# The rest of the keys' P is split into a rounded and a low part in the attention of a fused attention and two feed-forward layers

## The reference

```python
q_rot, k_rot = rotate(q), rotate(k)                      # [4, 8, 576, 64]
scores = (1 / sqrt(64)) * q_rot @ k_rot^T
attn = exp(scores - max); attn = attn / (sum(attn) + 1e-9)
x = (attn @ v) as [2304, 512]
h = x @ w_in;   x = (h - tanh(h)) @ w_out                # 512 -> 2048 -> 512
h = x @ w_in2;  out = (h * sigmoid(h)) @ w_out2
```

## Time and profile before

| | |
|---|---|
| median of three runs | 1110.88 us |
| the profiled execution's own time | 1111.94 us |
| its span, first to last instruction | 1110.1 us |
| mean granted TensorE clock | 1.000 |
| TensorE busy | 1075.9 us, 97% of the span |
| VectorE busy | 443.0 us, 40% |
| ScalarE busy | 419.5 us, 38% |
| GpSimd busy | 282.6 us, 25% |
| attention | up to 301 us of the span |
| feed-forward layers | from 301 us to the end |

### The profile page before, as it was taken

The page is one execution under the profiler, slowest core; times in us unless marked ns, Lnnn a source line. Parts: engine busy times, 40 slices in busy tenths (PEclk is TensorE's granted clock), DMA queues, the critical chain, the costliest instruction groups (busy, mean ns, idle before and its releaser), DMA issues.

```text
span 1110.1 us, 16519 instructions
## 1 busy us (share of the span) xinstructions
PE 1075.9 (97%) x6608; PEld 987.7 (89%) x6608; DVE 443.0 (40%) x712; ACT 419.5 (38%) x775; POOL 282.6 (25%) x121
## 2 busy tenths in 40 slices
PE   2899999999999999999999999999999999999998
PEld 1778888888899999999999999899999999899997
DVE  5566666666253323223232333623223232322322
ACT  1567686676722323223232322323223232232322
POOL 5776978873551000000000015700000000000000
PEclk9999999999999999999999999999999999999999
DMA  5344446532152000000000004200000000000000
GB/s 182 133 154 146 133 127 217 162 102 71 29 168 76 1 1 0 0 0 0 0 0 0 0 0 151 76 1 29 0 0 28 0 28 0 0 28 0 29 0 28
DMA packets 36331, 58.35 MB, mean 53 GB/s; under 512 B 15680, under 2 KB 17984, under 8 KB 34368
## 3 DMA queue, kind: packets, MB, share of 16 engines
q1 hardware_dynamic: 36288, 57.78, 16.0%
HBM read 48.37 MB, written 4.79 MB: 48 GB/s over the span
## 4 chain that ended last, share of the span: by engine, by line
PE 89%; POOL 5%; DVE 2%; DMA 1%; ACT 1%; issue 1%; SPq 0%; ACTq 0%; POOLq 0%; DVEq 0%
PE ps L597 35%; PE ps L616 18%; PE ps L611 17%; PE ps L535 6%; PE ps L501 4%; PE ps L466 2%; PE ps L530 2%; PE ps L527 1%; PE ps L503 1%; PE ps L493 1%; POOL wout_l L399 1%; POOL hl L379 1%; POOL win_l L399 1%; DVE hm L777 1%; POOL raw L374 1%
## 5 line engine op out<-in xcount | busy, mean ns | idle before, releaser
L597 PE MATMUL ps<-xs_h,win_l 128*128 128x384 f32 x768 | 258.6, 337 | 1.4 <-DVE xs_l L834 1.4
L597 PE MATMUL ps<-xs_h,win_h 128*128 128x384 f32 x768 | 257.6, 335 | 0.0
L597 PE MATMUL ps<-xs_l,win_h 128*128 128x384 f32 x768 | 257.1, 335 | 0.0
L742 ACT ACTIVATE g_h<-ps 128x384 fp32r<-128x384 f32 x192 | 94.5, 492 | 306.3 <-PE ps L616 135.1
L736 ACT ACTIVATE act<-ps 128x384 f32<-128x384 f32 x192 | 94.5, 492 | 247.6 <-PE ps L597 247.4
L597 PEld LDWEIGHTS ps<-xs_h,win_l 128*128 128x128 f32 x768 | 144.2, 188 | 7.5 <-issue 3.9
L597 PEld LDWEIGHTS ps<-xs_l,win_h 128*128 128x128 f32 x768 | 144.2, 188 | 3.5
L597 PEld LDWEIGHTS ps<-xs_h,win_h 128*128 128x128 f32 x768 | 144.1, 188 | 0.0
L777 DVE TENSOR_REDUCE hm<-ps 128x2 f32<-128x576 f32 x144 | 108.5, 756 | 79.8 <-PE ps L466 77.9
L399 POOL TENSOR_TENSOR win_l<-w_stage,win_h 128x2048 fp32r<-128x2048 f32 x8 | 39.6, 4953 | 350.2 <-DVE win_h L830 344.5
L611 PE MATMUL ps<-g_h,wout_h 128*128 128x384 f32 x384 | 128.3, 334 | 0.0
(11 more groups left out here) (75 smaller groups left out, 1523.5 us busy)
## 6 DMA issues: line engine op xcount, KB each, us to landing
raw<-qk SPq DMA_DIRECT2D x15, 1152.0 KB, 6.5
w_stage<-w_in SPq DMA_DIRECT2D x8, 1024.0 KB, 5.1
w_stage<-w_out SPq DMA_DIRECT2D x8, 1024.0 KB, 5.4
R<-inverse_sums SPq DMA_DIRECT2D x32, 144.0 KB, 3.1
v<-vfull SPq DMA_DIRECT2D x16, 256.0 KB, 2.9
out<-ostage SPq DMA_DIRECT2D x5, 768.0 KB, 3.6
vr<-vin SPq DMA_DIRECT2D x16, 192.0 KB, 3.2
ev<-ev SPq DMA_DIRECT2D x16, 144.0 KB, 2.3
```

Source lines behind the costliest of these rows:

```text
L597: last = mm(o, w[g][:, kk, c:c + 128], x[:, kk, :], start=(n == 0), stop=(n == 11))
L742: nc.scalar.activation(g_h[f % 2][:, :], ps[:, 4 + f % 4, 0:TN], ACT.Copy, scale=(1.0, 0.5)[L]).then_inc(s_gh, 1)
```

## The change

P of unit 2, the rest, is split as that of the other blocks is: it now gets a rounded part `ph[3]`, an in-place exponential and a low part `pl[3]`, in tiles of their own, and its V comes in the split form. It is weighed with three fp32r matmuls per head and query half instead of one float32 matmul. Two of nine units stay whole, those of block 3 (units 4 and 8). The tile `PR` goes. The load of V in split form grows from 192 to 256 KB, that in whole form shrinks from 256 to 128 KB. The wait for the whole V moves from the first half of unit 2 to unit 4.

```diff
-FULL = (3, REST)
-SPLIT = (0, 1, 2)
+FULL = (3,)
+SPLIT = (0, 1, 2, REST)
...
-        PR = place("PR", [128, 2, HALF])
-        ph = [place(f"ph{i}", [128, 2, HALF], F32R) for i in range(NS)]
-        pl = [place(f"pl{i}", [128, 2, HALF], F32R) for i in range(NS)]
-        v1 = [place(f"v1{i}", [128, 2, 2, 128]) for i in range(2)]
-        vh = [place(f"vh{i}", [128, 3, 2, 128], F32R) for i in range(2)]
-        vl = [place(f"vl{i}", [128, 3, 2, 128], F32R) for i in range(2)]
+        ph = [place(f"ph{i}", [128, 2, HALF], F32R) for i in range(NS + 1)]
+        pl = [place(f"pl{i}", [128, 2, HALF], F32R) for i in range(NS + 1)]
+        v1 = [place(f"v1{i}", [128, 1, 2, 128]) for i in range(2)]
+        vh = [place(f"vh{i}", [128, 4, 2, 128], F32R) for i in range(2)]
+        vl = [place(f"vl{i}", [128, 4, 2, 128], F32R) for i in range(2)]
...
         def ring(g):
-            return SPLIT_U.index(g % 9) % NS
+            return NS if g % 9 == 2 else [u for u in SPLIT_U if u != 2].index(g % 9) % NS
...
-                if half == 0:
+                if u == 4:
                     pe.wait_ge(s_vf[n % 2], 16 * (n // 2 + 1))
...
                 if i == REST:
-                    for h, a in enumerate(heads):
-                        last = mm(ps[:, OB + h, 0:HALF], v1[n % 2][a, 1, h, :], PR[a, half, :], start=first, stop=False)
+                    r, t = ring(g), SPLIT.index(i)
+                    for m, (w, x) in enumerate(((vh, pl), (vl, ph), (vh, ph))):
+                        for h, a in enumerate(heads):
+                            last = mm(ps[:, OB + h, 0:HALF], w[n % 2][a, t, h, :], x[r][a, half, :],
+                                      start=(first and m == 0), stop=False)
...
-                    nc.scalar.activation((PR if u == 2 else P)[:, :, :], s, ACT.Exp, scale=SCALE).then_inc(s_ex, 1)
+                    nc.scalar.activation(P[:, :, :], s, ACT.Exp, scale=SCALE).then_inc(s_ex, 1)
```

More of the change, by code:

```diff
@@ L85, in attention_and_two_ffn @@
         stab = place("stab", [128, 1, S])
-        vr = place("vr", [128, 3, 2, 64])
+        vr = place("vr", [128, 4, 2, 64])
         assert second_group_end <= cursor[0]
@@ L207, in ring @@
         def ring(g):
-            return SPLIT_U.index(g % 9) % NS
+            return NS if g % 9 == 2 else [u for u in SPLIT_U if u != 2].index(g % 9) % NS
         def place_of(g):
-            return -2 if g % 9 == 2 else -1 if is_full(g) else ring(g)
+            return -1 if is_full(g) else ring(g)
         def weighed(g):
```

## The result

The changed kernel takes 1120.74 us (median of four runs, 1119.83 to 1122.11), the kernel before 1111.47 us (four runs, 1110.35 to 1112.55). The ratio is 1.0084, its 95% interval 1.0067 to 1.0102: 9.3 us slower. The forecast was 1119.3 us, a loss of 8.4 us against the 1110.88 us that the kernel before had on record then.

The account below looks back on a forecast made before the run. TensorE, 97% busy, was taken as the bound, losing time by waits: pairs 4 to 14 7.0, pairs 1 to 3 1.8, first 0.1, pair 15 0.5, less 0.96 in pairs 5 and 8: 8.4 us, 1119.3 us; range 1115.5 to 1123.5.

Parts of the forecast that it names:

- Scores 4 are ready at 208.65 and would start at 209.23: Pair 10, TensorE: unit 4's scores wait for unit 2's low part to free their PSUM place, 0.58 us later.
- TensorE's wait: Unit 4's scores start late and run longer without preloaded weights, so the next `row_scores` comes 0.68 us later.
- VectorE's late maximum: Maximum queued behind unit 2's low part on VectorE; second `row_scores`, then unit 5's scores, come 0.73 us late.
- The rival of the bare wait: VectorE catches up, unit 5's scores are not held; 0.40 us a pair, 1116.3 us; chance 10%.
- the rival that adds it: ScalarE's extra 0.55 us per pair adds to VectorE's delay: 8.8 us more, 1128.1 us; chance 7%.
- The rival of halves that don't overlap: Two heads' fp32r matmuls of the rest queue up, each half 0.30 us longer: 1129.5 us; chance 6%.
- full passes: Alternative reading: float32 takes four full array passes, so each half of the rest gains 0.13 instead of 0.09 us.
- the one half that counts: Rest's second half, in the fifth step, gives its 0.09 us; the first half's is lost in the wait.
- Pairs 5 and 8: They already wait for unit 3's low part, so 0.48 us of the delay is swallowed in each.
- Pair 15: Already waits 0.99 us behind ScalarE; only ScalarE's 0.55 less 0.09 counts: 0.46 us longer.
- Pairs 1 and 2: With pair 3: third step's maximum 0.77 us late, both halves give 0.09, so 0.59 us longer each.
- The waits for `pl`: Sign: TensorE's waits for the low part sum to 8 us or more instead of 2.1.

Follow-up runs that it names:

- the wait alone: Kernel before, rest still weighed whole in float32, plus second exponential and an unread subtraction that unit 4's scores wait for: 1122.57 us, ratio 1.0102.
- the matmuls alone: Changed kernel without the rest's second exponential and subtraction, zeros standing for the low part: 1110.86 us, ratio 0.9998.
- the doubled subtraction: Changed kernel with the rest's subtraction done twice on VectorE, the first into an unread tile: 1132.50 us, ratio 1.0189.
- The early release: Changed kernel with the rest's unrounded exponential in SBUF, so unit 4's scores no longer wait for the subtraction: 1123.59 us, ratio 1.0114.
- VectorE's order alone: Changed kernel with only the rest's subtraction moved behind the third step's first maximum on VectorE: 1123.06 us, ratio 1.0106.
- The second exponential: Kernel before plus only the rest's second exponential, in place and unread, unit 4's scores waiting for it: 1114.78 us, ratio 1.0035.
- Both together: Changed kernel with unrounded exponential in SBUF, subtraction behind the third step's first maximum, unit 1 weighed before the rest's first half: 1117.33 us, ratio 1.0046.

## Why the prediction was right

- **The mechanism.** "Scores 4 are ready at 208.65 and would start at 209.23" and the queue behind it came out within 0.03 us at each of the six places of the table above. The run with the wait alone shows the loss without the new matmuls, the one with the matmuls alone shows no loss, and the doubled subtraction gives the slope: 0.68 us for 0.67.
- **The two delays that coincide.** The prediction gave TensorE's wait 0.68 us and VectorE's late maximum 0.73 and took the later. The early release takes the wait at unit 4 away and leaves the steady pair at 17.10 us, so VectorE's late maximum alone is enough for the whole loss. VectorE's order alone puts the maximum on time and leaves 17.51 us, but it makes the wait at unit 4 longer (0.99 us instead of 0.42), so it shows that such a wait costs and not how much the one of the changed kernel would by itself. With both and unit 1 weighed first the pair is 16.43; no run has that last move alone. The rival of the bare wait (1116.3 us) is excluded by the changed kernel's 0.67 a pair.
- **The second exponential** beside VectorE's delay: alone it costs 3.3 us, and the rival that adds it (1128.1 us) is excluded by the changed kernel's 0.67 per pair.
- **The new matmuls.** 0.56 us a half, from L501's row, is what L528 and L534 take. The rival of halves that don't overlap falls. Whether the gain would be 0.09 or 0.13 us (by full passes) is told by the wait-only run: its steady pair is 17.17, the changed one 17.08, 0.09 us for the one half that counts.
- **Pairs that differ.** Pairs 5 and 8 swallowed their share: 0.18 and 0.16 longer, 0.16 forecast. Pair 15: 0.47 against 0.46. Pairs 1 and 2: 0.64 and 0.67 against 0.59. The first: 0.02 against 0.1.
- **A sign that did not come out.** The waits for `pl` should have summed to 8 us or more; they sum to 6.3. The wait at unit 4 is 0.42 us and not about 0.5 in each of pairs 4 to 14, and pairs 1 to 3 have none there: they wait for the maximum, 1.08 us instead of 0.33, as the prediction's own paragraph on these pairs had it. Waits for maxima grew from 2.6 to 4.9 us. The sign counted one queue of the two.
- **What was mis-sized.** The sum was 8.4 us for pairs that measure 9.9. Of the difference 1.3 us is a term the prediction did not have, a fall of TensorE's clock behind a longer wait, in pair 3 of the profiled execution; the rest is 0.03 us for each steady pair. Two of the four runs, with the lower mean clock, are 1.7 us above the other two on average. That this wait brings the fall about is not shown: the same 1.08 us of idle time in pairs 1 and 2 had no fall behind them, the wait-only kernel fell behind the second of three such waits, and the kernel with the early release behind none. The longer idle time of 2.70 us had a fall behind it, and it went when the idle time went, in one profile each. Without the fall in pair 3 the pairs would be 8.6 us longer, closer to the 8.4 that were worked out.

## What to carry to other kernels

A resource that is freed later hurts in two places: at whoever waits for it, and behind the work that now stands in the freeing engine's queue. Work out the second from the distance of two starts on that engine before removing the first, since taking away one alone may bring nothing: here the early release brought nothing. A saving on an engine that has 97% of the span can be worth less than what it adds to the chains of the engines that feed it: here 0.18 us a pair against 0.73.

## What the runs showed of the hardware

A VectorE subtraction with both operands in SBUF took 0.75 us alone, and longer, up to 3.12 us, when a GpSimd instruction of 2.6 us on SBUF was running at its start. That was so in eleven cases over four kernels, and in each it ended 0.61 or 0.62 us behind the end of that instruction (39.65 against 39.03 in the one shown). With one operand in PSUM it took 0.74 us in the same place. The Trainium skill (SBUF — State Buffer, SBUF: two separate sides) says that VectorE with two SBUF inputs and a GpSimd instruction that reads SBUF hold a port pair one at a time, for a whole instruction; the rows agree. That makes a PSUM operand worth keeping where GpSimd is busy, as it is here for 163 of 222 us.

TensorE's granted clock went to half in some executions behind idle times of 1.1 to 2.8 us inside an otherwise full stream, for 3 to 7 us, and stayed up behind others as long (1.75 us in the kernel with the subtraction twice, 1.29 in that of "Both together"). One fall of 3 us cost pair 3 of the changed kernel 1.3 us. Runs of one kernel with such waits lay up to 7.5 us apart, those of the kernel before 2.9; that the falls make the spread is likely and not shown, since one execution of each kernel has a profile.
